# Sliding-window attention beside a dense network: attention blocks regrouped from six per stage in four stages to four per stage in six

## The chip, the cores and the metric

One core of a Trainium2 chip runs the whole program in one launch. The metric is the device time of that launch in microseconds (us), median of several executions. The engines are TensorE (PE in the profile, its weight loads PEld), VectorE (DVE), ScalarE (ACT), GpSimd (POOL) and the queue that issues most transfers, SyncE (SP). Each engine runs its instructions in order and waits on semaphores.

## What is computed

Three stages, cut to what matters:

```python
# q, k, v: (4, 8, 576, 64)   batch, heads, positions, head size
mask = (rel >= 0) & (rel < 64)               # each query sees 64 keys back
attn = softmax(where(mask, q @ k.T / 8, -1e9))
x = (attn @ v)                               # -> (2304, 512), rows by batch and position
h = ((x @ w1) * (x @ w2)) @ w3 @ w_out       # dense: 512 -> 1024 -> 1024 -> 512
e_idx = argmax(h @ w_gate)                   # one of 8 experts per row
out = gate * sigmoid(...) * relu(h @ ew1[e]) @ ew2[e]
```

## The kernel before, in words

Every large product is three products of fp32r parts: a high part and what the rounding left over (`product3`, L495 to L498: high x high, high x low, low x high). So each operand has a copy made by ScalarE (`h`) and a difference made by VectorE or GpSimd (`l`).

**Fold.** The kernel first multiplies w3 by w_out (and by the gates) into W, 512 + 16 columns, so that the dense part needs only w1, w2 and W. `w_order` lists its 16 tiles; the first two are done together in quarters. A W tile is 24 matmuls of 256 or 272 columns. Its result goes through ScalarE (`Wh`, L876) and VectorE (`Wl`, L1109). Beside that the fold splits w3 (`w3_steps`) and w1/w2 (`w12_steps`: at which tile each of eight pieces is copied by ScalarE; GpSimd makes the differences of the first six, L1463, and VectorE of the last two, `LATE`, L1065).

**Chunks.** The 2304 rows are six chunks of 384. `xTh` and `xTl` hold the transposed attention result of 1152 rows (two batches), three chunks. A chunk has 14 tiles, called steps e = 0 to 13: eight hidden tiles (w1 and w2, 24 matmuls of 384 columns) and six row tiles (24 matmuls against W, first three of 272 columns, then three of 256). The last chunk is followed by the routing and the experts, which the change leaves alone.

**Attention** has 24 blocks: a block is four heads by 192 queries (three groups of 64, each against 128 keys). They are put between the tiles of the stage before the chunk that needs them. A block passes through these pieces, each a function of the step after which it runs:
- `score` (TensorE, L587): 12 products into banks 5 and 7. It waits for q and k, and for the masks of the block before.
- `masks` (VectorE, `laid`): per head pair, scale and add the mask (L1021), take the maximum of two halves (L1025); then the row maximum (L1027).
- `exps` (ScalarE, `raised`, L830): six exponentials with sums.
- `weigh` (VectorE, `weighed`, L1045 and L1047) and `normal` (GpSimd, L1453): reciprocal, and the probabilities multiplied by it.
- `turn` (TensorE, `turned`, L599): three transposes into bank 4. It waits for `p_ok` of its block and for `pt_ok`, bank 4 read out for the block before.
- `turn_out` (VectorE, L1037): four copies out of bank 4, `pt_ok`.
- `value` (TensorE, `valued`, L612), `value_hi` (ScalarE, L835), `value_lo` (VectorE, L1051): product with v into bank 6, and its two parts into xTh and xTl. `value` waits for `o_lo`, the `value_lo` of the block before.

Before, a batch (six blocks) is done per stage, `NP` = 6, in four stages: in the fold, and in chunks 0, 2 and 3 (counted from 0); chunks 1, 4 and 5 have none. The blocks start every second step, and everything of one step runs in the order `turn`, `value`, `score` on TensorE. On VectorE, `weigh` stands inside the tile's own work, ahead of `turn_out`, `value_lo` and `masks` of the same step. The last block's `value` stands inside the last tile, behind nine of its matmuls:

```python
if b is not None and KF + i == NSTEP - 1:
    row_tile(i, n, tt, lambda: value(b, LAST))
```

**Transfers.** All loads are issued by the sync queue in an order written out by hand (up to L470). q and k of a block are two transfers into a buffer of a whole batch's two head pairs, v two more into tiles for even and odd starts. A load waits until the buffer's part was read (`next_qk`, `next_v`), and what stands behind it in the queue waits with it. Expert weights are loaded into the same room once the last block is done (`o_done`).

Of the kernel before, what the change touches and what calls it, by code (L numbers as in the profile page):

```python
# [18 lines left out]
P = 128  # L19
# [4 lines left out]
ALU = mybir.AluOpType  # L24
# [5 lines left out]
def build(nc, B, H, S, qT_in, kT_in, v_in, w1, w2, w3T_in, w_out, w_outT, w_gates, ew1, ew2, out):  # L30
    DM, FF = w1.shape
    D = DM // H
# [7 lines left out]
    SFULL = S // P  # L40
# [15 lines left out]
    UNITS = B * PAIRS  # L56
    UPS = 2 * PAIRS
# [7 lines left out]
    NP = PAIRS * NGRP // 2  # L65
    NSTEP = KF + 2 * CT
    assert 2 * NP + 2 == NSTEP and NCH == 3
# [4 lines left out]
    with ctx:  # L72
# [34 lines left out]
        put("raw_room", P)  # L107
# [110 lines left out]
        w12_hi, w12_lo, w1_lo = sem("w12_hi"), sem("w12_lo"), sem("w1_lo")  # L218

        qk_in, v_in_ok = [sem(f"qk_in{j}") for j in range(NGRP)], [sem(f"v_in{j}") for j in range(NGRP)]  # L220
# [15 lines left out]
        ew_hi, ew_lo = [sem("ew1_hi"), sem("ew2_hi")], [sem("ew1_lo"), sem("ew2_lo")]  # L236
# [15 lines left out]
        def v_tile(r, i):  # L252
            t = vA if key_start(i) % P == 0 else vB
            c = key_start(i) // P * 2 + r
            return t[:, c * P:(c + 1) * P]

        v_tiles = [[sorted({key_start(i) // P for i in range(3 * j, 3 * j + 3) if key_start(i) % P == odd * WIN})
                    for j in range(NGRP)] for odd in range(2)]
        unit_of = lambda p: divmod(p, NGRP)
# [41 lines left out]
        def pair_x(t, p, parity):  # L301
            u, j = unit_of(p)
            c = parity * S + j * 3 * WIN
            return t[:, :].rearrange("p (k c) -> p k c", c=SUPER)[:, 2 * u:2 * u + 2, c:c + 3 * WIN]
# [18 lines left out]
        def fold_scored(i):  # L323
            return i - 2 if i in (2, 3) else scored(i - 2) if i > 3 else None

        def fold_laid(i):
            return i - 2 if i in (2, 3) else laid(i - 2) if i > 3 else None

        def fold_raised(i):
            return 0 if i == 2 else raised(i - 2) if i > 3 else None  # L330

        def fold_weighed(i):
            return weighed(i - 2) if i > 2 else None
# [5 lines left out]
        w12_steps = [3, 6, 8, 10, 11, 12, 13, 14]  # L339
        LATE = 2 * KD - 2  # L340
# [43 lines left out]
        def _(sp):  # L384
# [33 lines left out]
            def load_qk(u, j):  # L418
                cols = slice(j * 3 * WIN, (j + 1) * 3 * WIN)
                for t, src in ((qT, qT_in), (kT, kT_in)):  # L420
                    sp.dma_start(t[:, :].rearrange("p (r s) -> p r s", s=S)[:, :, cols],
                                 src[bass.ds(u * 2, 2), :, cols].rearrange("r p s -> p r s")).then_inc(qk_in[j], 16)

            def load_v(u, j):
                for odd, vt in enumerate((vA, vB)):
                    t0, t1 = v_tiles[odd][j][0], v_tiles[odd][j][-1] + 1
                    sp.dma_start(vt[:, t0 * 2 * P:t1 * 2 * P].rearrange("p (t c) -> p t c", c=2 * P),
                                 v_in[bass.ds(u, 1), odd * WIN + t0 * P:odd * WIN + t1 * P, :].rearrange("o (t p) c -> p (o t) c", p=P)
                                 ).then_inc(v_in_ok[j], 16)

            def next_qk(u, j):
                sp.wait_ge(s_done, u * (2 * NGRP) - (2 * NGRP) + min(2 * j + 4, 2 * NGRP))
                load_qk(u, j)

            def next_v(u, j):
                sp.wait_ge(o_done, u * NGRP - NGRP + j + 1)
                load_v(u, j)

            load_qk(0, 0)
            for i in range(KF // 2):  # L440
                load_wo(1, i)
            load_qk(0, 1)
            load_qk(0, 2)
            load_v(0, 0)
            load_w12(0)
            load_v(0, 1)
            load_w12(1)
            load_v(0, 2)
            next_qk(1, 0)
            load_w3(4)  # L450
            next_qk(1, 1)
            next_qk(1, 2)
            load_w12(2)
            load_w3(6)
# [1124 lines left out]
```

## Time and profile before

| | |
|---|---|
| median of 3 runs | 717.49 us (716.71 to 718.61) |
| profiled execution, its own time | 718.94 us |
| its span, first to last instruction | 717.2 us |
| instructions | 15001 |
| mean granted clock of TensorE | 0.995 of full speed |
| busy VectorE, ScalarE, GpSimd | 378.0, 268.5, 119.9 us |
| q and k, each of 24 transfers of 192 KB | 3.0 and 4.0 us to landing |
| fold, chunks, and rest | to 84 us, to 437, to 717 |

The span is what the trace's rows add up to; the 1.7 us between it and the execution's time lie around it. In a timeline a row's second number is the duration of one instruction or of a merged group. TensorE's matmuls overlap, so the step from one to the next (start to start) is what counts there, and it is shorter than the duration. "idle before <-" names what ended an idle time.

### The profile page before, as it was taken

What the parts mean: (1) busy time and instruction counts of PE and PEld (TensorE: products, weight loads), DVE (VectorE), ACT (ScalarE), POOL (GpSimd) and SP (SyncE); (2) the same over time, 40 slices, a digit from 0 to 9 for tenths busy, and PEclk for the clock granted to TensorE, in tenths of its full rate; (3) what the DMA queues carried; (4) which work ended last, traced back from release to release, by engine and by line L of the source; (5) the groups of instructions that cost most, each with busy time, mean ns of one, the idle gap of its engine ahead of it and who ended that gap; (6) DMA issues with size and microseconds to landing.
All of it is one profiled execution on the core that took longest, in us unless ns stands there. A gap on an engine that the chain in (4) does not pass through costs nothing.

```text
span 717.2 us, 15001 instructions
## 1 busy us (share of the span) xinstructions
PE 701.5 (98%) x5075; PEld 639.1 (89%) x5076; DVE 378.0 (53%) x711; ACT 268.5 (37%) x651; POOL 119.9 (17%) x179
## 2 busy tenths in 40 slices
PE   8999899999999999999999999999999999999997
PEld 7999799999999989999999999878888888888885
DVE  5789657732237755782222568845356554662211
ACT  4466244322124324432211254444446444552121
POOL 7224200100010010001000001222222122222211
PEclk9999899999999999999999999999999999999999
DMA  9875121320012242115201043746265753511110
GB/s 328 273 263 175 45 67 39 111 82 1 4 64 60 66 138 75 29 36 199 81 1 45 1 127 126 262 161 216 75 224 187 234 173 133 183 35 44 32 44 30
DMA packets 44590, 80.12 MB, mean 112 GB/s; under 512 B 4413, under 2 KB 24893, under 8 KB 44544
## 3 DMA queue, kind: packets, MB, share of 16 engines
q1 hardware_dynamic: 39504, 64.01, 27.3%
q0 software_dynamic: 5040, 15.47, 6.2%
q8 instruction: 32, 0.52, 0.3%
q14 instruction: 14, 0.11, 0.0%
HBM read 70.03 MB, written 10.49 MB: 112 GB/s over the span
## 4 chain that ended last, share of the span: by engine, by line
PE 91%; DVE 4%; DMA 1%; issue 1%; ACT 1%; POOL 1%; POOLq 0%; DVEq 0%; ACTq 0%
PE bank L496 27%; PE bank L498 26%; PE bank L497 26%; PE bank L771 3%; PE bank L587 3%; PE bank L612 2%; DVE pT L1037 2%; PE bank L749 1%; PE bank L599 1%; DMA xs<-x_rows,gidc 1%; DVE prob L1025 1%; PE bank L509 1%; PE bank L731 1%; DMA w3r<-in_w3T 1%; DVE w3l L1058 1%
## 5 line engine op out<-in xcount | busy, mean ns | idle before, releaser
L496 PE MATMUL bank<-Wh,abh 128*128 128x272 f32 (+1 forms) x288 | 83.5, 290 | 0.0
L498 PE MATMUL bank<-Wh,abl 128*128 128x272 f32 (+1 forms) x288 | 82.1, 285 | 0.0
L1128 DVE TENSOR_TENSOR wbuf<-raw,wbuf 128x1024 f32 (+1 forms) x64 | 75.3, 1220 | 12.5 <-ACT wbuf L896 12.4
L497 PE MATMUL bank<-Wl,abh 128*128 128x272 f32 (+1 forms) x288 | 81.9, 284 | 0.0
L1329 DVE TENSOR_TENSOR hTl<-bank,hTh 128x512 fp32r<-128x512 f32 x44 | 28.4, 685 | 97.9 <-ACT hTh L944 90.5
L1149 DVE TENSOR_TENSOR ab_f<-bank,a_sb 128x384 f32<-128x384 f32 x48 | 26.7, 555 | 94.2 <-PE bank L498 93.7
L496 PE MATMUL bank<-wbuf,hTh 128*128 (+1 forms) x176 | 70.7, 402 | 0.6 <-issue 0.6
L496 PE MATMUL bank<-wbuf,xsTh 128*128 (+1 forms) x176 | 70.5, 400 | 0.0
L498 PE MATMUL bank<-wbuf,hTl 128*128 (+1 forms) x176 | 68.8, 391 | 0.0
L497 PE MATMUL bank<-wbuf,xsTh 128*128 (+1 forms) x176 | 68.7, 390 | 0.0
L498 PE MATMUL bank<-wbuf,xsTl 128*128 (+1 forms) x176 | 68.6, 390 | 0.0
L497 PE MATMUL bank<-wbuf,hTh 128*128 (+1 forms) x176 | 68.4, 389 | 0.0
L904 ACT ACTIVATE abh<-ab_f 128x384 fp32r<-128x384 f32 x48 | 25.2, 525 | 111.8 <-DVE ab_f L1149 111.8
L496 PE MATMUL bank<-xTh,w1h 128*128 128x384 f32 x192 | 66.0, 344 | 0.0
L497 PE MATMUL bank<-xTl,w1h 128*128 128x384 f32 x192 | 64.2, 335 | 0.0
L498 PE MATMUL bank<-xTh,w1l 128*128 128x384 f32 x192 | 64.2, 334 | 0.0
L498 PE MATMUL bank<-xTh,w2l 128*128 128x384 f32 x192 | 64.2, 334 | 0.0
L496 PE MATMUL bank<-xTh,w2h 128*128 128x384 f32 x192 | 64.1, 334 | 0.0
L497 PE MATMUL bank<-xTl,w2h 128*128 128x384 f32 x192 | 64.1, 334 | 0.0
L896 ACT ACTIVATE wbuf<-raw 128x1024 f32 (+1 forms) x64 | 63.9, 1054 | 0.0
L1037 DVE TENSOR_TENSOR pT<-bank,side 64x384 f32<-64x384 f32 x96 | 53.1, 554 | 12.7 <-PE bank L599 11.3
L496 PEld LDWEIGHTS bank<-Wh,abh 128*128 128x128 f32 x288 | 54.2, 188 | 1.1 <-issue 0.5
(218 smaller groups left out, 1479.9 us busy)
## 6 DMA issues: line engine op xcount, KB each, us to landing
raw<-in_expert_w SPq DMA_DIRECT2D x64, 512.0 KB, 4.4
qT<-in_qT SPq DMA_DIRECT2D x24, 192.0 KB, 3.0
kT<-in_kT SPq DMA_DIRECT2D x24, 192.0 KB, 4.0
x_rows<-x_sb POOLq DMA_DIRECT2D x18, 256.0 KB, 2.3
w3r<-in_w3T SPq DMA_DIRECT2D x8, 512.0 KB, 6.2
wo<-in_w_out SPq DMA_DIRECT2D x8, 256.0 KB, 8.0
woT<-in_w_outT SPq DMA_DIRECT2D x4, 512.0 KB, 8.3
vA<-in_v SPq DMA_DIRECT2D x16, 128.0 KB, 2.2
```

What stands on the lines that cost most here:

```text
L496: pe.matmul(dst, lh, rh, start=first, stop=False)
L497: pe.matmul(dst, lh, rl, start=False, stop=False)
L498: return pe.matmul(dst, ll, rh, start=False, stop=last)
L587: mm = pe.matmul(score_bank(h)[r * WIN:(r + 1) * WIN, (i % 3) * P:(i % 3 + 1) * P], qT[rows, r * S + i * WIN:r * S + (i + 1) * WIN], kT[ro ...
L612: mm = pe.matmul(bank[6][r * D:(r + 1) * D, (3 * h + i) * WIN:(3 * h + i + 1) * WIN], v_tile(r, 3 * j + i)[:, h * D:(h + 1) * D], pT[buf_o ...
L771: mm = pe.transpose(bank[3 + n][:, (f % 4) * P:(f % 4 + 1) * P], h_sb[:, f * P:(f + 1) * P], ident[:, :])
L896: act.activation(wbuf[:, bass.ds(wcol(e, part, 0, c * PC), PC)], raw[part * NP1 + c][:, :], ACT.Copy).then_inc(ew_hi[part], 1)
L904: act.activation(abh[:, f * CH:(f + 1) * CH], ab_f[f % 2][:, :], ACT.Copy).then_inc(ab_hi, 1)
L1037: cut = dve.tensor_tensor(pT[buf_of(p, h)][w * WIN:(w + 1) * WIN, :].rearrange("p (i r c) -> p i r c", r=2, c=WIN), bank[4][rows, 0:3 * P] ...
L1128: dve.tensor_tensor(wbuf[:, bass.ds(wcol(e, part, 1, c * PC), PC)], raw[part * NP1 + c][:, :], f32(wbuf[:, bass.ds(wcol(e, part, 0, c * PC ...
L1149: dve.tensor_tensor(ab_f[f % 2][:, :], hidden_bank(cc, f, 1)[:, 0:CH], a_sb[f % 2][:, :], ALU.mult).then_inc(ab_ok, 1)
L1329: dve.tensor_tensor(hTl[last][:, cols], bank[3 + n][:, :], f32(hTh[last][:, cols]), ALU.subtract).then_inc(hT_lo, 1)
```

## The change

The 24 blocks are ordered as the chunks need them: of each pair of batches, first the blocks of the first 384 rows (both halves of the heads), then of the next 384, then of the last. `NP` becomes 4, and every stage but the last chunk has attention: the fold and chunks 0 to 4. q and k of a block are one transfer of 448 KB, v one of 384 KB, each into one of two buffers by the block's parity; the host lays them out block by block (keys that two blocks share are stored twice). The steps at which pieces run are given as tables. In `masks` the two maxima are one instruction over both head pairs. Of the differences of w1 and w2, GpSimd now makes three (pieces 2, 4, 5) and VectorE five, and two of the steps at which they are copied change. The sync queue has no loop left for attention; in each stage it issues the loads of blocks two to five ahead.

```diff
+def pair_order(B, H):
+    order = []
+    for si in range(B // 2):
+        for stage in (((0, 0), (0, 1)), ((0, 2), (1, 0)), ((1, 1), (1, 2))):
+            order += [(2 * si + half, u, j) for u in range(H // 4) for half, j in stage]
+    return order
...
-    NP = PAIRS * NGRP // 2
+    PLACES = pair_order(B, H)
+    STAGES = NSUP * NCH
+    NP = len(PLACES) // STAGES
...
-        qT, kT = put("qT", 2 * S), put("kT", 2 * S)
-        vA, vB = put("vA", 2 * SFULL * P), put("vB", 2 * SFULL * P)
-        sm = put("sm", 3 * P)
+        qk = [put(f"qk{i}", QK) for i in range(2)]
+        vv = [put(f"vv{i}", 6 * P) for i in range(2)]
+        sm = put("sm", 2 * 3 * P)
...
         def scored(e):
-            return e // 2 + 1 if e % 2 == 0 and e // 2 + 1 < NP else None
+            return {2: 1, 5: 2, 8: 3}.get(e)
+
+        def laid(e):
+            return {0: 0, 3: 1, 6: 2, 9: 3}.get(e)
+
+        def raised(e):
+            return {1: 0, 4: 1, 7: 2, 9: 3}.get(e)
+
+        def weighed(e):
+            return {2: 0, 5: 1, 8: 2, 10: 3}.get(e)
 
         def turned(e):
-            return e // 2 - 1 if e % 2 == 0 and e >= 2 else None
+            return {4: 0, 7: 1, 10: 2, 11: 3}.get(e)
 
         def valued(e):
-            return e // 2 - 2 if e % 2 == 0 and e >= 4 else None
-
-        def laid(e):
-            return (e + 1) // 2 if e % 2 and (e + 1) // 2 < NP else None
-
-        def raised(e):
-            return e // 2 if e % 2 == 0 and e // 2 < NP else None
-
-        def weighed(e):
-            return e // 2 if e % 2 and e // 2 < NP else None
+            return {6: 0, 9: 1, 12: 2}.get(e)
...
-                batches = si * 2 + (1 if c == 0 else 2)
-                b = None if c == 1 or final else batches
-                chunk(cc, c, batches, b, 1 if c == 0 else 0, final)
+                chunk(cc, c, None if final else cc + 1, final)
...
         def fold_scored(i):
-            return i - 2 if i in (2, 3) else scored(i - 2) if i > 3 else None
+            return 0 if i == 2 else scored(i - 2)
...
-        w12_steps = [3, 6, 8, 10, 11, 12, 13, 14]
-        LATE = 2 * KD - 2
+        w12_steps = [3, 6, 8, 9, 10, 12, 13, 14]
+        w12_pool = (2, 4, 5)
...
+            def load_qk(G):
+                if G >= 2:
+                    sp.wait_ge(s_done, 2 * (G - 1))
+                sp.dma_start(qk[G % 2][:, :], qk_pairs[G]).then_inc(qk_in[G % 2], 16)
+
+            def load_v(G):
+                if G >= 2:
+                    sp.wait_ge(o_done, G - 1)
+                sp.dma_start(vv[G % 2][:, :], v_pairs[G]).then_inc(v_in[G % 2], 16)
+
+            load_qk(0)
             for i in range(KF // 2):
                 load_wo(1, i)
+            load_qk(1)
+            load_v(0)
             load_w12(0)
+            load_v(1)
+            load_qk(2)
             load_w12(1)
             load_w3(4)
+            load_qk(3)
+            load_w3(6)
             load_w12(2)
             load_w3(5)
             load_w12(3)
             load_w12(4)
+            load_qk(4)
             load_w12(5)
+            load_v(2)
+            load_w3(7)
             load_w12(6)
+            load_qk(5)
             load_w12(7)
+            load_v(3)
+            load_v(4)
+            load_v(5)
+            for G in range(NP, len(PLACES), NP):
+                for load, ahead in ((load_qk, 2), (load_qk, 3), (load_qk, 4), (load_v, 2),
+                                    (load_qk, 5), (load_v, 3), (load_v, 4), (load_v, 5)):
+                    if G + ahead < len(PLACES):
+                        load(G + ahead)
...
                 for h in range(2):
-                    g = 2 * G + h
-                    dve.wait_ge(s_done, g + 1)
-                    if g > 0:
-                        dve.wait_ge(laid_ok, g)
-                    dve.scalar_tensor_tensor(sm[:, :], score_bank(h)[:, 0:3 * P], SEQ_SCALE,
+                    dve.wait_ge(s_done, 2 * G + h + 1)
+                    dve.scalar_tensor_tensor(sm[:, h * 3 * P:(h + 1) * 3 * P], score_bank(h)[:, 0:3 * P], SEQ_SCALE,
...
-                    dve.wait_ge(masked, g + 1)
-                    dve.tensor_tensor(pr[:, :, h, :], smv[:, :, 0, :], smv[:, :, 1, :], ALU.max).then_inc(laid_ok, 1)
-                dve.wait_ge(laid_ok, 2 * G + 2)
+                dve.wait_ge(masked, 2 * G + 2)
+                smv = sm[:, :].rearrange("p (h i w c) -> p h i w c", h=2, w=2, c=WIN)
+                dve.tensor_tensor(prob[p % 2][:, :].rearrange("p (i h c) -> p h i c", h=2, c=WIN),
+                                  smv[:, :, :, 0, :], smv[:, :, :, 1, :], ALU.max).then_inc(laid_ok, 1)
+                dve.wait_ge(laid_ok, G + 1)
...
-                if b is not None:
-                    masks(b, 0)
                 for f in range(KF):
```

The last cut is in VectorE's `chunk`: block 0's masks stood ahead of the first hidden tile's work there and now follow it (`laid` of step 0).

## Rows read from the trace of the kernel before

**Rows 1.** The page, busy us of the engines (share of the span) and instructions.
```profile
PE 701.5 (98%) x5075; PEld 639.1 (89%) x5076; DVE 378.0 (53%) x711; ACT 268.5 (37%) x651; POOL 119.9 (17%) x179
```

**Rows 2.** The waits of TensorE: line, releaser, us in total, times, longest us.
```profile
PE bank L599 <- POOL prob L1453: 4.6, 4, 3.4
```

**Rows 3.** Windows by stage: us, busy us by engine, granted clock, DMA share, GB/s.
```profile
84.08:149.96 65.88, 64.84 (x644) 61.70 (x644) 43.68 (x96) 23.84 (x97) 6.25 (x8) 1.00 0.26 77
149.96:200.89 50.93, 50.93 (x339) 50.80 (x337) 10.44 (x22) 9.30 (x19) 1.62 (x3) 1.00 0.06 21
75.20:82.03 6.83, 6.14 (x61) 5.36 (x61) 2.97 (x6) 1.43 (x2) 0.54 (x1) 0.50 0.23 60
```

**Rows 4.** The timeline of TensorE, first chunk: start us, us, engine, line, operation.
```profile
120.82 0.44 PE L496 MATMUL bank<-xTh,w1h 128*128 128x384 f32 x1
...
123.00 0.33 PE L496 MATMUL bank<-xTh,w2h 128*128 128x384 f32 x1
...
125.08 0.28 PE L496 MATMUL bank<-Wh,abh 128*128 128x272 f32 x1
...
128.35 0.52 PE L599 MATMUL bank<-ident,prob 128*128 128x128 f32 x3
...
130.47 0.39 PE L496 MATMUL bank<-Wh,abh 128*128 128x272 f32 x1
...
136.62 0.49 PE L599 MATMUL bank<-ident,prob 128*128 128x128 f32 x3
137.04 0.45 PE L612 MATMUL bank<-pT,vA 128*64 128x64 f32 x8
...
137.89 0.39 PE L496 MATMUL bank<-Wh,abh 128*128 128x256 f32 x1
...
143.68 0.49 PE L599 MATMUL bank<-ident,prob 128*128 128x128 f32 x3
...
146.00 0.28 PE L498 MATMUL bank<-Wh,abl 128*128 128x256 f32 x1
...
147.22 0.28 PE L612 MATMUL bank<-pT,vB 128*64 128x64 f32 x2 [0.95 <-DVE xTl L1051]
```

**Rows 5.** The timeline of TensorE in the fold.
```profile
27.62 0.89 PE L587 MATMUL bank<-kT,qT 64*64 64x128 f32 x24
...
28.76 0.36 PE L496 MATMUL bank<-xTh,w3h 128*128 128x272 f32 x1 [0.25 <-DVE wol L1073]
```

**Rows 6.** The timeline of ScalarE, first chunk.
```profile
138.40 0.34 ACT L830 ACTIVATE prob<-prob,nmx 128x64 f32<-128x64 f32 x1
...
140.30 0.19 ACT L830 ACTIVATION_READ_ACCUMULATOR prob<-prob,nmx 128x1 f32 x1
...
145.07 0.49 ACT L835 ACTIVATE xTh<-bank 128x384 fp32r<-128x384 f32 x1 [0.80 <-PE bank L612]
```

**Rows 7.** The timeline of VectorE, first chunk.
```profile
86.65 0.36 DVE L1025 TENSOR_TENSOR prob<-sm 128x192 f32<-128x192 f32 x1
87.04 0.55 DVE L1027 TENSOR_REDUCE nmx<-prob 128x6 f32<-128x384 f32 x1
...
134.22 0.16 DVE L1045 TENSOR_SCALAR sums<-sums 128x6 f32<-128x6 f32 x1
...
134.52 0.53 DVE L1021 SCALAR_TENSOR_TENSOR sm<-bank,mask 128x384 f32<-128x384 f32 x1
...
140.52 0.17 DVE L1045 TENSOR_SCALAR sums<-sums 128x6 f32<-128x6 f32 x1
...
144.21 2.28 DVE L1037 TENSOR_TENSOR pT<-bank,side 64x384 f32<-64x384 f32 x4 [3.29 <-PE bank L599]
...
146.52 0.56 DVE L1051 TENSOR_TENSOR xTl<-bank,xTh 128x384 fp32r<-128x384 f32 x1
```

**Rows 8.** The timeline of VectorE in the fold.
```profile
65.82 1.76 DVE L1025 TENSOR_TENSOR prob<-sm 128x192 f32<-128x192 f32 x1
...
73.87 1.19 DVE L1065 TENSOR_TENSOR w1l<-w1r,w1h 128x1024 fp32r<-128x1024 f32 x1
```

More of the change, by code:

```diff
@@ L27, with build @@
 NEG = -1.0e30
-def build(nc, B, H, S, qT_in, kT_in, v_in, w1, w2, w3T_in, w_out, w_outT, w_gates, ew1, ew2, out):
+def pair_order(B, H):
[4 more added lines that the diff above has]
+    return order
+def build(nc, B, H, S, qk_pairs, v_pairs, w1, w2, w3T_in, w_out, w_outT, w_gates, ew1, ew2, out):
     DM, FF = w1.shape
@@ L106, in build @@
         mask, side = put("mask", 4 * P), put("side", 2 * 4 * WIN)
-        put("raw_room", P)
+        put("raw_room", 6 * P)
         attn_end = put.o
@@ L250, in key_start, with key_offset @@
             return WIN * max(i - 1, 0)
[L252 to L259, printed above, removed]
+        def key_offset(j, i):
+            return key_start(3 * j + i) - key_start(3 * j)
+        head_of_row = lambda G: PLACES[G][2] == 0
         score_bank = lambda h: bank[5 + 2 * h]
@@ L323, in fold_scored @@
         def fold_scored(i):
-            return i - 2 if i in (2, 3) else scored(i - 2) if i > 3 else None
[L326 to L333, printed above, removed]
+            return 0 if i == 2 else scored(i - 2)
         w3_steps = {1: 3, 5: 4, 7: 5, 9: 6, 11: 7}
-        w12_steps = [3, 6, 8, 10, 11, 12, 13, 14]
-        LATE = 2 * KD - 2
+        w12_steps = [3, 6, 8, 9, 10, 12, 13, 14]
+        w12_pool = (2, 4, 5)
+        pool_count = lambda n: sum(i in w12_pool for i in range(n))
         assert len(w12_steps) == 2 * KD
@@ L463, in _ @@
             load_w12(7)
-            next_v(1, 2)
-            with sp.Fori(2, UNITS // 2) as u:
-                for j in range(NGRP):
-                    next_qk(u, j)
-                for j in range(NGRP):
-                    next_v(u, j)
+            load_v(3)
[6 more added lines that the diff above has]
+                        load(G + ahead)
@@ L578, in score @@
                 G = b * NP + p
-                u, j = unit_of(p)
-                pe.wait_ge(qk_in[j], (b * (PAIRS // 2) + u + 1) * (16 * 2))
+                j, buf = PLACES[G][2], qk[G % 2]
+                pe.wait_ge(qk_in[G % 2], 16 * (G // 2 + 1))
                 if G > 0:
                     pe.wait_ge(masked, 2 * G)
-                for i in range(3 * j, 3 * j + 3):
+                for i in range(3):
                     for h in range(2):
@@ L887, in _ @@
                     hi_wo(1)
-                if fold_raised(i) is not None:
-                    exps(0, fold_raised(i))
+                if raised(i - 2) is not None:
+                    exps(0, raised(i - 2))
                 if i in w12_steps:
@@ L1032, in turn_out @@
                 rows = slice(h * WIN, (h + 1) * WIN)
-                lead = 0 if unit_of(p)[1] == 0 else 1
+                lead = 0 if head_of_row(G) else 1
                 dve.wait_ge(pt_done, G + 1)
@@ L1109, in own @@
                     dve.tensor_tensor(Wl[:, ws], w_bank(i)[:, 0:end - first], f32(Wh[:, ws]), ALU.subtract).then_inc(W_lo, 1)
-                    if fold_weighed(i) is not None:
-                        weigh(0, fold_weighed(i))
+                    if weighed(i - 2) is not None:
+                        weigh(0, weighed(i - 2))
                 if i == len(w_order) - 1:
-                    value_lo(0, LAST, 0)
+                    value_lo(0, LAST)
                 own()
@@ L1119, in _ @@
                 if i >= 2 and valued(i - 2) is not None:
-                    value_lo(0, valued(i - 2), 0)
-                if fold_laid(i) is not None:
-                    masks(0, fold_laid(i))
+                    value_lo(0, valued(i - 2))
+                if laid(i - 2) is not None:
+                    masks(0, laid(i - 2))
             weight_splits(len(w_order) - 1)
@@ L1180, in chunk @@
                     if b is not None and KF + i == NSTEP - 1:
-                        value_lo(b, LAST, parity)
+                        value_lo(b, LAST)
                     row_tile(i, n, tt)
@@ L1462, in lo_w12 @@
                 pool.wait_ge(w12_hi, i + 1)
-                pool.tensor_tensor(wl[:, ws], wr[:, ws], f32(wh[:, ws]), ALU.subtract).then_inc(w12_lo, 1)
+                pool.tensor_tensor(wl[:, ws], wr[:, ws], f32(wh[:, ws]), ALU.subtract).then_inc(w12_lo_pool, 1)
             for i in range(len(w_order)):
-                if fold_weighed(i) is not None:
-                    normal(0, fold_weighed(i))
-                if i in w12_steps[:LATE]:
+                if weighed(i - 2) is not None:
+                    normal(0, weighed(i - 2))
+                if i in w12_steps and w12_steps.index(i) in w12_pool:
                     lo_w12(w12_steps.index(i))
```

120 lines of the change are left out of this document (44 added, 76 removed).

## The prediction

> **What bounds the kernel now.** I read the page's busy times first: TensorE is busy 701.5 us of a span of 717.2 [rows 1]. Whatever the change does to other engines counts only through TensorE: how much it has to issue, where it waits, and at which clock it runs. Then the waits of TensorE: four waits of `turn` (L599) for GpSimd's normalisation, 4.6 us in all, the longest 3.4 [rows 2]; all lie in the fold, where attention runs between the products of w3 and w_out. Then the windows by stage [rows 3]. A chunk without attention takes 50.93 us and TensorE has no idle time in it; the chunk with six blocks takes 65.88. VectorE is busy 43.68 us in the one and 10.44 in the other, so a block costs VectorE about 5.5 us, and the DMA engines are at 0.26. The third window, just behind the 3.4 us wait, has a granted clock of 0.50, that is 1.2 GHz in place of 2.4, with TensorE busy for 6.14 us of it.
>
> Last, TensorE's own timeline through a chunk with attention [rows 4]. Start to start, the twelve matmuls of w1 behind a `score` take 2.18 us and the next twelve 2.08: the first piece behind attention costs 0.10 more. Two row tiles of 272 columns take 6.15 us behind attention, so 3.03 each plus 0.10 once; two of 256 columns take 5.79, so 2.85 each plus 0.10. A `turn` takes 0.42 us, a `value` 0.85. The first row tile takes 3.27, with 0.25 more than it needs, spent on the normalisation. The last `value` starts 1.22 us behind the ninth matmul of its tile where 0.12 is the step: 1.1 us of waiting.
>
> **Part 1: attention is spread over six stages of four blocks.** All 24 blocks remain, with the same matmuls, so their own time only moves (two blocks out of the fold, two out of each chunk that had six, four into each that had none). What changes is the number of places at which tiles are interrupted. By the schedule functions a stage has 9 such places before (start, after 0, 2, 4, 6, 8, 10, 12, and inside the last tile), in four stages: 36. After, it has 12 (start, after 2, 4, 5, 6, 7, 8, 9, 10, 11, 12, inside the last), in six stages: 72. At 0.10 us each, 36 more add **3.6 us**; the bounds are 0, should the step hide behind weight loads, and 0.13.
>
> In the fold, `score` 1 no longer stands behind the fourth tile. Before, it ran at 27.62 and TensorE then waited 0.25 us for the low part of the gate columns until 28.76 [rows 5]. Nothing stands in its place, so all of that 1.1 us is idle: **+0.85 us**, since the block's work comes later anyway.
>
> **Part 2: the waits that go.** `weighed` and `turned` are now two tiles apart for blocks 0 to 2 where they were one, so normalisation is done long before it is asked for: the four fold waits go, **-4.6** [rows 2], and with the longest the half clock behind it, 6.14/2 = **-3.1** [rows 3]. In three chunks the 0.25 us behind the first row tile go, **-0.75**, and the wait of the last `value`, 3 x 1.1 = **-3.3** [rows 4], because no `turn_out` stands before `value_lo` any more. What remains of it: `value` 3 needs the low half of `value` 2, which is 0.97 us from the start of a `value` to ScalarE's copy (144.10, which is `turn` at 143.68 and 0.42, to 145.07), 0.52 for the copy, 0.56 for the subtraction and 0.14 to TensorE (147.08 to 147.22) [rows 4, 6, 7], together 2.19, against 0.85 + 0.10 + 9 x 0.119 = 2.02 of TensorE's work: 0.17 us in five chunks, **+0.85**.
>
> **Part 3: the new wait.** Block 3 is the tight one. Its mask is made after tile 9, its exponentials follow, its sums are taken after tile 10, block 2 is turned out only behind them on VectorE, and `turn` 3 on TensorE after tile 11 waits until block 2 is out of bank 4. Before, two turns stood two tiles apart; now these two are one apart.
> From the end of tile 9, TensorE has `value` 1 0.85, tile 10 3.13, `turn` 2 0.42, tile 11 2.95: 7.35 us.
> The other chain: 0.97 and 0.52 as above; `value_lo` 0.50; the masks, now two scale-and-mask steps, one maximum over 384 columns and one reduction; 0.03 to ScalarE; the exponentials 2.12 (138.40 to 140.52); sums and reciprocal 0.30 (134.22 to 134.52); `turn_out` 2.28 and 0.14 to TensorE [rows 6, 7]. The masks I put at 0.53 + 0.53 for the two steps, 0.56 and 0.55 for maximum and reduction with 0.03 before each, 2.2 in all: the wide maximum is in no row, 192 columns take 0.36 and two of these 0.72, I take 0.56. Sum 9.1 us, a wait of **1.75 us**, 1.55 to 1.9 by those bounds. Queued behind the waiting `weigh` on VectorE is nothing but this `turn_out`. Five chunks: **+8.8**.
> In the fold the same chain holds one more copy on ScalarE and one more subtraction on VectorE, of tile 12, each narrower than the 0.49 and 0.56 of 384 columns [rows 6, 7]: 0.4 each. A w1 split on GpSimd can lie beside the maximum; in the fold a maximum beside one took 1.76 us in place of 0.36 [rows 7, 8], so 0 to 1.4 more, and I take 0.2, as they meet only at the edge. That makes 2.7 us there (2.3 to 4.1): **+2.7**.
>
> **Part 4: what I cost at nothing.** Three of six splits of w1/w2 go from GpSimd to VectorE, 3 x 1.2 us of VectorE [rows 8], against two blocks fewer, 2 x 5.5 us [rows 3]: the fold's VectorE is freer than before, and only a backlog longer than a tile would reach TensorE. The merged maxima shorten VectorE's masks; they are in the chain above and nowhere else. The two transfers of a block are 448 and 384 KB, in place of 384 and 256 to 384. On the sync queue each load waits for the block two before it and is asked for at least three tiles later, over 9 us. Load 2 now stands before w2's second piece, load 3 before w3's seventh, load 4 and `v` 2 before later pieces of w1: each wait ends on a block that TensorE has done three or more tiles before the piece is due. With the DMA engines at 0.26 in a chunk this is covered; if the cover fails, TensorE stands for the whole missing part. The expert weights' first loads wait for block 24, now at the end of the fifth chunk, and are needed behind the eight hidden tiles of the sixth, 33 us on.
>
> **Sum.** Gone: 4.6 + 3.1 + 3.3 + 0.75 = 11.7. New: 3.6 + 0.85 + 0.85 + 8.8 + 2.7 = 16.8. Net +5.1 us on the span of 717.2. The profiled execution itself took 718.94, 1.45 above the median of 717.49; I add the difference to the median: **722.6 us**. The largest single gain, 7.7 us in the fold, is real, and is paid back because one wait now comes six times.
>
> **Rivals.** (a) The fold's new wait brings the clock down. A wait of 3.4 us did so before, ones of 1.1 did not [rows 2 to 4]; 2.7 lies between. Price 3.1 us: 725.7, slower still. Chance 0.17; against it, the point estimate is below the one wait that did it. The Trainium skill, "TensorE: Matmul & The Clock Gate", section "Why this matters for your kernels", warns that idle gaps between bursts of matmuls bring the half clock back; by it this rival is the danger of any schedule with one long wait, and the trace agrees with its 6.14 us at 0.50.
> (b) Not slower: block 3's chain closes in time. If it reaches TensorE within 7.35 us after tile 9, the 8.8 and 2.7 vanish: 711.1. It needs 1.75 us out of ScalarE's exponentials and VectorE's order, for instance if `turn_out` 2 ran before `weigh` 3. The code gives weights first, so 0.10.
> (c) The waits are there, but the interruptions cost nothing and the wait is at its lower bound: 722.6 - 3.6 - 1.0 = 718.0, no change. 0.12.
> (d) A load comes late in the fold, or VectorE's backlog reaches TensorE there: 3 to 5 us more, 727. 0.08.
> The forecast itself: 0.53.
>
> **How the numbers follow.** A measurement tells 0.3% from nothing, that is 2.2 us. Faster is (b); same is (c); slower is the forecast, (a) and (d). The range from 718 to 727.5 leaves out (b) and part of (d).
>
> **What would show it.** TensorE's waits should list `turn` behind VectorE's `turn_out`, six times, about 1.7 us each and one near 2.7, and none behind GpSimd. Chunks one to five should each take about 50.93 + 4 x 2.09 + 1.2 + 1.9 = 62.4 us, where 2.09 is a block's own matmuls (0.42, 0.85 and some 0.82 of a `score`, whose 0.89 overlaps the next [rows 5]). The fold should end about 8 us earlier. I am wrong if the chunks take 60.5 (the wait is hidden), or if the granted clock shows a dip in each chunk, or if a DMA is named in TensorE's waits.

## The result, and the profile after

The changed kernel takes 724.88 us (median of four, 723.52 to 725.88) against 717.71 for the kernel before beside it: a ratio of 1.0099, interval 1.0077 to 1.0121. It is slower, inside the forecast range of 718 to 727.5 and 2.3 us above the forecast.

The page of the kernel after, head and busy row, answers to [rows 1]:

```profile
span 721.8 us, 14724 instructions
...
PE 702.3 (97%) x5075; PEld 638.6 (88%) x5076; DVE 368.0 (51%) x690; ACT 268.2 (37%) x651; POOL 113.6 (16%) x176
```

VectorE and GpSimd have 10.0 and 6.3 us less to do than in [rows 1], TensorE 0.8 more, and the span is 4.6 us longer. So 3.8 us of it were lost while TensorE stood, and 0.8 while it worked. Its waits, where [rows 2] had GpSimd's normalisation (line 583 is now `turn`, 1016 `turn_out`):

```profile
engine line waited for: us in total, times, longest us
PE bank L583 <- DVE pT L1016: 10.8, 6, 2.7
PE bank L557 <- DVE prob L1060: 1.5, 1, 1.5
PE bank L479 <- DVE wol L1052: 1.1, 1, 1.1
```

The waits for GpSimd are gone and so are the three of the last `value` for its low half. In their place stands one new kind, six times: `turn` for `turn_out` of the block before, 2.7 us in the fold and 1.6 in each of five chunks. The third line is the gate columns' wait: 1.1 us with nothing before it, where [rows 5] had 0.25. No DMA is in the list.

Windows of the kernel after (us, busy us by engine, granted clock, DMA share, GB/s, as in [rows 3]): the first, second and fifth chunk, and the stretch behind the fold's wait:

```profile
77.26:139.72 62.46, 60.81 (x542) 58.09 (x541) 31.30 (x68) 19.01 (x71) 4.66 (x6) 1.00 0.21 62
139.72:202.18 62.46, 60.82 (x542) 58.10 (x541) 30.61 (x66) 19.00 (x71) 4.99 (x7) 1.00 0.23 68
327.10:389.42 62.32, 60.67 (x541) 58.09 (x541) 30.61 (x66) 19.00 (x71) 4.98 (x7) 1.00 0.16 49
...
67.60:70.90 3.30, 3.30 (x18) 3.30 (x16) 2.88 (x6) 0.00 (x0) 0.69 (x1) 0.50 0.02 5
```

All five chunks with attention take 62.3 to 62.5 us, of which 1.65 is TensorE idle (62.46 less 60.81). The first chunk begins at 77.26 where it began at 84.08: the fold gains 6.8. The sixth begins at 389.42; before, chunks of 65.88 and 50.93 brought it there at 383.53, so the chunks lose 12.7 (312.16 against 299.45). What follows takes 332.4 against 333.6: there the profile of the kernel before has two waits of TensorE that this one has not, 0.6 us at 468.25 with no releaser in the profile and 0.4 at 467.01 for the gathered rows. The three make up the span: -6.8 + 12.7 - 1.3 = +4.6. The two rows of the kernel before:

```profile
467.01 0.66 PE L749 MATMUL bank<-ident,xs 128*128 128x128 f32 x4 [0.36 <-DMA xs<-x_rows,gidc]
468.25 0.49 PE L496 MATMUL bank<-wbuf,hTh 128*128 x1 [0.58 <-issue]
```

One wait in TensorE's timeline, first chunk after the change (columns as in [rows 4]): the tile after `turn` 2, and the wait at `turn` 3:

```profile
126.43 0.49 PE L583 MATMUL bank<-ident,prob 128*128 128x128 f32 x3
126.68 0.36 PE L479 MATMUL bank<-Wh,abh 128*128 128x256 f32 x1
...
129.49 0.28 PE L481 MATMUL bank<-Wh,abl 128*128 128x256 f32 x1
131.40 0.55 PE L583 MATMUL bank<-ident,prob 128*128 128x128 f32 x3 [1.63 <-DVE pT L1016]
```

From the tile's last matmul to the `turn` is 1.91 us where one step is 0.12: TensorE loses 1.79. What it waits for, in VectorE's timeline of the same stretch:

```profile
123.95 0.56 DVE L1030 TENSOR_TENSOR xTl<-bank,xTh 128x384 fp32r<-128x384 f32 x1 [0.88 <-ACT xTh L817]
124.43 1.01 DVE L998 SCALAR_TENSOR_TENSOR sm<-bank,mask 128x384 f32<-128x384 f32 x2
125.47 0.56 DVE L1003 TENSOR_TENSOR prob<-sm 128x384 f32<-128x384 f32 x1
126.07 0.55 DVE L1006 TENSOR_REDUCE nmx<-prob 128x6 f32<-128x384 f32 x1
...
128.79 0.17 DVE L1024 TENSOR_SCALAR sums<-sums 128x6 f32<-128x6 f32 x1 [1.65 <-ACT prob L812]
128.99 0.19 DVE L1026 RECIPROCAL rec<-sums 128x6 f32<-128x6 f32 x1
129.10 2.24 DVE L1016 TENSOR_TENSOR pT<-bank,side 64x384 f32<-64x384 f32 x4
```

`turn` 2 is in the bank at 126.9, and VectorE is idle for 1.65 us until 128.79, yet `turn_out` 2 starts only at 129.10: ahead of it in VectorE's order stands `weigh` 3, which waits for block 3's exponentials, and these for the masks made after tile 9. That is the chain of part 3 of the prediction. The wide maximum, which no row showed before, takes 0.56.

### The profile page after: what moved, and what is told of

The parts are those of the page before. It is cut to its first block, busy times and chain, and to the rows that moved or that the text cites. A ratio compares the mean times of both kernels' runs of the same rounds, so it can differ in the third digit from the quotient of the medians.

```text
span 721.8 us, 14724 instructions
## 1 busy us (share of the span) xinstructions
PE 702.3 (97%) x5075; PEld 638.6 (88%) x5076; DVE 368.0 (51%) x690; ACT 268.2 (37%) x651; POOL 113.6 (16%) x176
## 4 chain that ended last, share of the span: by engine, by line
PE 91%; DVE 5%; ACT 2%; issue 1%; DMA 1%; POOLq 0%; ACTq 0%; DVEq 0%
PE bank L479 27%; PE bank L481 25%; PE bank L480 25%; PE bank L595 3%; PE bank L571 3%; PE bank L753 3%; DVE pT L1016 2%; ACT prob L812 2%; PE bank L731 1%; PE bank L583 1%; DVE sm L998 1%; PE bank L492 1%; DVE prob L1003 1%; PE bank L713 1%; DMA w3r<-in_w3T 1%
## 5 line engine op out<-in xcount | busy, mean ns | idle before, releaser
L479 PE MATMUL bank<-Wh,abh 128*128 128x272 f32 (+1 forms) x288 | 85.4, 297 | 0.0
L1430 POOL TENSOR_TENSOR prob<-prob,rec 128x384 f32<-128x384 f32 x24 | 20.8, 867 | 286.6 <-DVE rec L1026 286.6
```

The costliest lines, as they stand in the source:

```text
L479: pe.matmul(dst, lh, rh, start=first, stop=False)
L1430: pool.tensor_tensor(pv, pv, rec[:, stats(p)].unsqueeze(2).broadcast_to([P, 6, WIN]), ALU.mult).then_inc(p_ok, 1)
```

## The experiments

All were timed beside the kernel before (717.2 to 718.2 us in their sessions) on one core. To compare two of them, take the difference of their ratios; 0.1% is 0.7 us. They add lines to the program, so the same code has other line numbers in some of them.

| kernel | us | ratio to before | interval |
|---|---|---|---|
| the change | 724.88 | 1.0099 | 1.0077 to 1.0121 |
| chunks_block3_early | 716.30 | 0.9983 | 0.9973 to 0.9994 |
| fold_retimed | 718.58 | 1.0015 | 1.0005 to 1.0024 |
| turn_out_first | 721.01 | 1.0051 | 1.0032 to 1.0071 |
| fold_wait_filled | 722.64 | 1.0076 | 1.0059 to 1.0093 |
| chunks_grouped | 713.79 | 0.9952 | 0.9934 to 0.9969 |
| best | 707.72 | 0.9871 | 0.9849 to 0.9893 |
| before_three_splits_moved | 717.91 | 1.0005 | 0.9995 to 1.0015 |
| two_maxima | 725.32 | 1.0114 | 1.0097 to 1.0131 |
| loads_twice | 724.17 | 1.0086 | 1.0070 to 1.0103 |
| gpsimd_six_splits | 723.84 | 1.0077 | 1.0060 to 1.0094 |

### Block 3 one tile earlier in the chunks

The fold keeps the change's tables; the chunks get:

```diff
 def scored(e):
-    return {2: 1, 5: 2, 8: 3}.get(e)
+    return {2: 1, 5: 2, 7: 3}.get(e)
 def laid(e):
-    return {0: 0, 3: 1, 6: 2, 9: 3}.get(e)
+    return {0: 0, 3: 1, 6: 2, 8: 3}.get(e)
 def raised(e):
-    return {1: 0, 4: 1, 7: 2, 9: 3}.get(e)
+    return {1: 0, 4: 1, 7: 2, 8: 3}.get(e)
```

> The changed kernel, with block 3's score, masks and exponentials one step earlier in the five chunks (score after step 7, masks and exponentials after step 8) and the fold left as it is. Theory (the wait of turn 3 for bank 4 is what the change costs): turn_out 2 is then ready before TensorE has done tile 11, the wait of 1.8 us goes in all five chunks, each chunk takes 60.6 us in place of 62.45, and the time falls by 9 us, to 715.9 (from 724.9, the kernel before at 717.7). Rival (the twelve interruptions of every stage cost it, not the wait): their number stays at twelve, and the time stays at 724 to 725. The fold's wait of 2.7 us stays under both.

716.30 us. Waits and first chunk of this kernel:

```profile
PE bank L589 <- DVE pT L1027: 2.7, 1, 2.7
```
```profile
78.51:139.19 60.68, 60.67 (x541) 58.06 (x540) 31.17 (x68) 18.87 (x71) 4.65 (x6) 1.00 0.20 65
```

The five short waits are gone and the fold's is left. A chunk takes 60.68, so 1.78 less, and TensorE is busy for all of it. Three table entries are worth 1.16%, more than the whole loss: without the wait of `turn` 3 in the chunks the change would not have been slower. One thing more differs: with `score` 3 behind `turn` 1 a chunk has eleven places of interruption and not the twelve that the expectation speaks of; by the prediction's price that is 0.1 us of the 1.78.

### VectorE's order at that place

```diff
 def weights(e):
-    if b is not None and weighed(e) is not None:
+    if b is not None and weighed(e) is not None and e != 10:
         weigh(b, weighed(e))
 def attend(e):
     if b is not None and turned(e) is not None:
         turn_out(b, turned(e), 0)
         turn_out(b, turned(e), 1)
+    if b is not None and e == 10:
+        weigh(b, weighed(e))
```

> The changed kernel; in the chunks VectorE turns block 2 out of bank 4 before it takes block 3's sums at step 10, nothing else. Theory: bank 4 is free 3.1 us after tile 10 ends and TensorE needs it at 3.4, so the wait for bank 4 goes; in its place the normalisation of block 3 comes late by some 0.9 us, since its sums now follow turn_out. The wait shrinks from 1.8 to about 0.9 us and changes its releaser from VectorE to GpSimd: 4 us faster, 721. Rival (the exponentials alone set the wait, whatever the order on VectorE): no change, 724.9.

721.01 us. Waits of this kernel, the two of `turn`:

```profile
PE bank L583 <- POOL prob L1432: 5.2, 5, 1.0
...
PE bank L583 <- DVE pT L1016: 2.7, 1, 2.7
```

With `turn_out` 2 ahead, bank 4 is free in time, and `turn` 3 waits 1.0 us for its own probabilities instead: a chunk takes 61.85, 0.6 less. So VectorE's order was the last link, but block 3's chain through exponentials, sums and normalisation is late by itself. So rival (b)'s remedy gives back a third of a chunk's 1.78 us, and the earlier block 3 all of it.

### The fold

The same idea in the fold alone, chunks as changed. It also puts `score` 1 back behind the gate columns' tile:

```diff
-            return 0 if i == 2 else scored(i - 2)
+            return 0 if i == 2 else {1: 1, 4: 2, 6: 3}.get(i - 2)
+fold_laid = {0: 0, 2: 1, 5: 2, 6: 3}.get
+fold_raised = {2: 0, 4: 1, 5: 2, 8: 3}.get
+fold_weighed = {2: 0, 5: 1, 7: 2, 8: 3}.get
+fold_turned = {4: 0, 6: 1, 10: 2, 11: 3}.get
+fold_valued = {6: 0, 10: 1, 11: 2}.get
```

> The changed kernel with the fold's steps retimed and the chunks left as they are: blocks 1 to 3 are scored one or two steps earlier (block 1 again behind the fourth tile, where it hides the wait for the gate columns), the sums of block 3 are taken at step 8. Theory: both fold waits (1.1 for the gates, 2.7 for bank 4) go, and with the second the half clock behind it. By durations alone the fold ends 4.1 us earlier; without the half clock 1.7 us more for a stretch of 3.4 us at 1.2 GHz, 3.4 us more for one of 6.8. Time 718 to 719.5. Rival: the half clock has another cause, then only 4.1 us go (720.8) and a stretch at 0.5 stays in the fold. The chunks' five waits of 1.8 us stay under both.

718.58 us, 0.84% below the change. Waits of this kernel, and its fold as one window:

```profile
PE bank L589 <- DVE pT L1027: 8.1, 5, 1.6
```
```profile
0.00:71.42 71.42, 69.27 (x661) 64.27 (x662) 48.35 (x87) 37.54 (x99) 26.97 (x51) 1.00 0.67 248
```

Only the chunks' five waits are left, there is no half clock in the fold, and it ends at 71.42 in place of 77.26. The 5.8 us are the 2.9 by which the wait holds TensorE up (below), some 0.9 of the gate columns', 1.7 of half clock (below) and 0.4 more. These tables also interrupt the fold at seven places where the change's do at twelve; at the prediction's 0.10 that would be 0.5, an estimate that no run takes apart.

### The half clock behind the fold's wait

TensorE's timeline in the fold after the change, at the wait:

```profile
64.28 0.28 PE L481 MATMUL bank<-xTl,w3l 128*128 128x272 f32 x1
67.28 0.71 PE L583 MATMUL bank<-ident,prob 128*128 128x128 f32 x3 [2.71 <-DVE pT L1016]
67.64 0.56 PE L479 MATMUL bank<-xTh,w3h 128*128 128x256 f32 x1
...
70.77 0.37 PE L481 MATMUL bank<-xTl,w3l 128*128 128x256 f32 x1
70.97 0.29 PE L479 MATMUL bank<-xTl,w3h 128*128 128x256 f32 x1
...
72.14 0.92 PE L595 MATMUL bank<-pT,vv 128*64 128x64 f32 x24
```

Behind 2.7 us of idleness a matmul of 256 columns takes 0.41 us in place of 0.28 until 70.8, at a granted clock of 0.50 (the last window above), 1.2 GHz in place of 2.4. The tile lasts 4.50 us (67.64 to 72.14) where its like lasts 2.93 (126.68 to 129.61 in the first chunk): with 0.12 in the `turn` 1.7 us are lost. The wait itself holds TensorE up for 2.88 us, 64.28 to 67.28 less a step of 0.12. Rival (a) happened, at half its price. To separate the idleness from the work behind it, this kernel fills the wait, with no result used:

```diff
 def turn(b, p):
+    if G == 3:
+        pe.wait_ge(masked, 8)
+        for _ in range(16):
+            pe.matmul(bank[7][:, 0:P], ident[:, :], ident[:, :], start=True, stop=True)
```

> The changed kernel with 16 extra matmuls (identity by identity, 128 columns, into bank 7, their result is read by nobody) put ahead of turn 3 in the fold, so that TensorE works through most of its wait of 2.7 us. No work of the reference is changed. Theory (the idle wait brings the half clock): no stretch at 0.5 in the fold, the extra matmuls cost nothing, the time falls by 1.7 to 3.4 us, to 721.5 to 723.2. Rival (the half clock comes from elsewhere or costs nothing): the stretch stays and the time is 724.9 or more.

722.64 us, by the ratios 0.23% below the change. The intervals of the two overlap, so the times alone do not settle it; the granted clock does. Two windows of its profiled execution, an early stretch and the one behind `turn` 3:

```profile
28.32:31.74 3.42, 2.95 (x13) 2.98 (x14) 1.07 (x5) 2.86 (x13) 0.00 (x0) 0.50 0.02 5
67.00:72.00 5.00, 5.00 (x46) 5.00 (x45) 4.05 (x8) 0.94 (x1) 2.77 (x2) 1.00 0.01 3
```

Behind `turn` 3 the clock stays at 1.00. The three executions beside this one ran at a mean clock of 0.999, which leaves some 2 us of half clock at most in the whole program, so no stretch of 3.4 us (worked out from span and mean clock). All seven profiles of the changed fold in which the wait was left idle have it. So it was the idleness. But this execution has a half clock that I did not expect, right behind the gate columns' wait of 1.1 us, and it was the slowest of its four (724.36; the others 722.54 to 722.68, so about 1.7 us for the stretch, as above). chunks_block3_early (28.16 to 31.57) and two_maxima (29.62 to 33.03) show the same stretch; the profile of the change, with the same wait, does not.

### What freed the fold: the schedule or the lighter GpSimd

The kernel before, with pieces 2, 4 and 5 of the w1/w2 differences on GpSimd and five on VectorE, and nothing else:

```diff
-        LATE = 2 * KD - 2
+        w12_pool = (2, 4, 5)
...
-                if i in w12_steps[LATE:]:
+                if i in w12_steps and w12_steps.index(i) not in w12_pool:
```

> The kernel before, six blocks per stage, with one part of the change alone: of the differences of w1 and w2, GpSimd makes pieces 2, 4 and 5 and VectorE the other five. It asks what freed the fold: the schedule (normalisation is asked for two tiles later) or GpSimd's lighter load. Theory (the schedule): the four waits of turn for the normalisation stay, since normalisation is still asked for one tile after the sums, and with them the half clock: 716.5 to 718.5, no change; the longest wait may shrink from 3.4 us to some 2.2 because GpSimd has one split less ahead of it, and VectorE's 3 x 1.2 us are covered. Rival (the split beside it made them): the waits fall to under 1 us in all and the half clock goes, 710.5 to 712.

717.91 us, 1.0005: no change. Waits of this kernel, and the window behind the longest:

```profile
PE bank L600 <- POOL prob L1453: 4.4, 3, 3.4
PE bank L613 <- DVE xTl L1051: 2.8, 3, 0.9
```
```profile
75.73:79.15 3.42, 3.29 (x31) 2.87 (x32) 2.29 (x5) 0.89 (x2) 0.00 (x0) 0.51 0.00 0
```

One wait less, the longest still 3.4 and the half clock still behind it, 3.42 us of it where the profile of before had 6.83. So it was not the splits but the new schedule that freed the fold; that it was the two tiles between `weighed` and `turned` is argued from the code and was not tried alone. The other way round, the change with GpSimd's six splits back:

```diff
-        w12_pool = (2, 4, 5)
+        w12_pool = (0, 1, 2, 3, 4, 5)
```

> The changed kernel with the first six differences of w1 and w2 on GpSimd again and two on VectorE, as before the change; all else as changed. Theory (a split of GpSimd beside VectorE's masks slows them, and the fold's turn 3 hangs on those masks): the fold's wait of turn 3 grows from 2.7 us to some 3.5, the chunks stay at 62.4, and the half clock behind it lasts longer: 725.5 to 727.5. Rival (the work taken off GpSimd did nothing): 724.9, wait 2.7.

723.84 us, not above the change. The mechanism is there, the price is not. Waits and VectorE's maximum in its fold, then the same maximum in the fold of the change:

```profile
PE bank L583 <- DVE pT L1016: 11.4, 6, 3.3
...
60.29 1.60 DVE L1003 TENSOR_TENSOR prob<-sm 128x384 f32<-128x384 f32 x1
```
```profile
60.32 1.00 DVE L1003 TENSOR_TENSOR prob<-sm 128x384 f32<-128x384 f32 x1
```

GpSimd's split lies beside the maximum for 1.18 us here (until 61.47) and for 0.59 in the change (until 60.91). The maximum runs 0.6 us longer and the wait is 0.6 longer. In this profile the half clock began at 67.33 (window below), half a microsecond before `turn` 3 was let go at 67.85: what of it falls into the wait costs nothing, so the tile behind took 4.06 us in place of 4.50. Moving three splits was worth nothing in either kernel.

```profile
67.33:70.74 3.41, 2.89 (x14) 2.89 (x15) 2.79 (x6) 0.00 (x0) 1.54 (x1) 0.50 0.00 0
```

### The merged maxima and the transfers

The maximum head pair by head pair again:

```diff
-                dve.wait_ge(masked, 2 * G + 2)
-                dve.tensor_tensor(prob[p % 2][:, :].rearrange("p (i h c) -> p h i c", h=2, c=WIN),
-                                  smv[:, :, :, 0, :], smv[:, :, :, 1, :], ALU.max).then_inc(laid_ok, 1)
+                for h in range(2):
+                    dve.wait_ge(masked, 2 * G + h + 1)
+                    dve.tensor_tensor(pr[:, h], smv[:, h, :, 0, :], smv[:, h, :, 1, :], ALU.max).then_inc(laid_ok, 1)
```

> The changed kernel with the maximum of a block made head pair by head pair again, 192 columns each, in place of one over 384. It leads to the exponentials of block 3 on the chain that sets turn 3. Before, 192 columns took 0.36 us. In the chunks VectorE has the second pair's scores as soon as the first, so two of them take 0.72 + a gap where one takes 0.56 to 0.7: theory (the chain through the masks sets turn 3): every wait of turn 3 grows by 0.1 to 0.3 us, 725.5 to 726.5, and the waits of TensorE at turn rise from 13.5 us to 14.1 to 15.3. Rival (masks are not on that chain): unchanged at 724.9, waits unchanged at 13.5.

725.32 us, 0.15% above, inside both intervals. The waits of `turn`, and VectorE at block 3 in its first chunk:

```profile
PE bank L583 <- DVE pT L1017: 10.7, 6, 2.9
```
```profile
126.22 1.01 DVE L998 SCALAR_TENSOR_TENSOR sm<-bank,mask 128x384 f32<-128x384 f32 x2
127.15 0.62 DVE L1005 TENSOR_TENSOR prob<-sm 128x192 f32<-128x192 f32 x2
127.81 0.55 DVE L1007 TENSOR_REDUCE nmx<-prob 128x6 f32<-128x384 f32 x1
```

My expectation failed. Two narrow maxima take 0.62 and not 0.72 plus a gap. From the first mask step to the reduction is 1.59 us here (126.22 to 127.81) and 1.64 with one wide maximum (124.43 to 126.07). A chunk takes 62.40 against 62.46. Merging gives nothing. That masks are on the chain stands by the experiment before: there the fold's wait grew by what the maximum did. It did here too: in the fold the two narrow ones take 1.25 us beside the split where the wide one took 1.00, and the wait is 2.9.

Every load of blocks 6 to 23 made twice, the second after the first has landed:

```diff
 sp.dma_start(qk[G % 2][:, :], qk_pairs[G]).then_inc(qk_in[G % 2], 16)
+if G >= 6:
+    sp.wait_ge(qk_in[G % 2], 16 * (2 * (G // 2) - 2))
+    sp.dma_start(qk[G % 2][:, :], qk_pairs[G]).then_inc(qk_in[G % 2], 16)
```

> The changed kernel with every load of q and k and of v for blocks 6 to 23 made twice into the same buffer, the second issued when the first has landed. TensorE waits for the second. A load is so twice as many bytes and comes a landing time later (3.2 us for q and k, 3.5 for v in the changed kernel's trace), and the queue stands for that time. Theory (the loads of the chunks are hidden; a load has three tiles, over 9 us, of room): 724.9 within 0.8, no DMA in TensorE's waits. Rival (the room is used up, the transfers are part of the time): each block late by a few tenths to 3 us, 730 or more, with waits of TensorE for a DMA at the score or the value in each chunk.

724.17 us, the same as the change. Its second chunk, to be held against the window 139.72:202.18 above:

```profile
140.42:202.86 62.44, 60.81 (x545) 58.09 (x541) 30.60 (x66) 18.98 (x71) 4.98 (x8) 1.00 0.39 122
```

The DMA share goes from 0.23 to 0.39 and the chunk stays at 62.4, with no DMA in TensorE's waits. The loads of the chunks are hidden with at least one landing time to spare. This says nothing of the loads of the fold, which were left as they were.

### Fewer places, and both together

The early block 3 with its pieces put between fewer tiles, first alone, then with the retimed fold:

```diff
 def turned(e):
-    return {4: 0, 7: 1, 10: 2, 11: 3}.get(e)
+    return {5: 0, 7: 1, 10: 2, 11: 3}.get(e)
 def valued(e):
-    return {6: 0, 9: 1, 12: 2}.get(e)
+    return {7: 0, 10: 1, 11: 2}.get(e)
```

> The chunks of chunks_block3_early, with the same pieces put between fewer tiles: turn 0 moves from behind tile 4 to behind tile 5 (where score 2 is), value 0 behind tile 7 (with turn 1 and score 3), value 1 behind tile 10 (with turn 2), value 2 behind tile 11 (with turn 3). A chunk has 7 places at which its tiles are interrupted in place of 11; the work is the same and the fold is untouched. Theory (an interruption costs 0.10 us, and the last value waits 0.17 us for the low half of the block before): 5 x 4 x 0.10 + 5 x 0.17 = 2.85 us less than chunks_block3_early's 716.3, so 713.4, and chunks of 60.1 to 60.2 us in place of 60.7. Rival (the time belongs to the pieces and not to the places, so grouping them gives nothing): 715.5 to 716.3, chunks of 60.5 to 60.7. A wait of a turn for a value's bank or of a value for its operands would add to either and would show in TensorE's waits.

> The chunks of chunks_grouped and the fold of fold_retimed together. If the gains add: the changed kernel's 724.9, less 8.6 for block 3 earlier in the chunks, 2.9 for grouping, and 6.3 for the fold (724.9 - 718.6) = 707.1. Rival (the fold and the chunks are coupled: block 4's load and masks, or the state in which the fold leaves VectorE, take back part of it): 709 to 711, with a wait of TensorE in the first chunk or for a DMA. By the theory the fold keeps five short waits of turn of about 1.6 us and the chunks have none over 0.3.

713.79 and 707.72 us. The first chunk of chunks_grouped, then waits and first chunk of best:

```profile
77.28:137.52 60.24, 60.24 (x541) 58.03 (x541) 31.14 (x68) 19.10 (x71) 4.66 (x6) 1.00 0.19 65
```
```profile
PE bank L563 <- DVE prob L1071: 1.5, 1, 1.5
PE bank L531 <- DVE wol L1063: 0.9, 1, 0.9
...
72.29:132.54 60.25, 60.25 (x544) 58.04 (x540) 30.62 (x67) 19.09 (x71) 4.69 (x7) 1.00 0.19 67
```

Grouping gives 0.44 us a chunk, where I expected 0.57. The wait of the last `value` had less than the expected 0.17 us to give: that `value` starts 0.29 behind the last matmul in chunks_block3_early (136.11 to 136.40) and 0.21 here (134.51 to 134.72), as any `value` does that waits for nothing. So 0.08 is the wait and four places fewer give 0.36, near the 0.40 expected. In best no `turn`, `value` or `score` is left among TensorE's waits. One line of its expectation was wrong by my own slip: it said the fold would keep five waits of 1.6 us, but those lay in the chunks and are gone with them. The gains add: 724.88, less 8.6, 2.5 and 6.3 for the three steps, is 707.5, and 707.72 was measured. This version beats both kernels, the one before by 1.3% (0.9849 to 0.9893).

## Why the prediction was right, by its steps

**What bounds it.** TensorE does: VectorE has ten us less to do and the kernel is slower, by TensorE's waits, its clock and its interruptions.

**The new wait (+8.8 in the chunks, +2.7 in the fold).** This step decided, and its chain holds the right links: 1.79 us measured for 1.75, and 2.88 for 2.7. Taking it away in the chunks brought 8.6 us back. That the size came out so near is in part luck. The chain took 8.94 us (122.46 to 131.40), not 9.1 (the terms as written add up to 9.06), as `turn_out` and the way from it to TensorE were 0.12 shorter; TensorE's own work beside it took 7.15, not 7.35, mostly because a `turn` that stands alone takes 0.25 us and not 0.42. The two errors cancel. In the fold the maximum took 1.00 us, not 0.56 and the 0.2 allowed for the split beside it; the other terms of the chain came out shorter, 9.98 us in all for 10.1, and TensorE's own work took 7.10.

**What went.** The 4.6 us of waits for GpSimd went, and before_three_splits_moved and gpsimd_six_splits show that it was by the schedule. So did the 0.25 us behind the first row tile: `turn` 1 now stands ahead of that tile, and it lasts 3.19 (115.23 to 118.42) with both its places, where it took 3.27. The last `value`'s 3.3 went too; by the forecast's measure 0.18 us of it is left (136.91 in the first chunk, 0.30 behind the last matmul, less a step of 0.12), forecast at 0.17. Half of that is no wait: a `value` that waits for nothing starts 0.21 behind the last matmul (134.50 to 134.71).

**The half clock (-3.1).** This is the term that failed. I let it go whole; 3.4 us of it came back behind the 2.7 us wait, and rival (a), to which I gave 0.17, is what happened, with 1.7 us lost and not 3.1. It is also why the fold ends 6.8 us earlier and not about 8. My argument against it, that 2.7 lies below the one wait that had done it, was no argument: the nearest row on the other side was at 1.1, and a wait of 1.1 too, that of the gate columns, is followed by the half clock in some executions. The Trainium skill, "TensorE: Matmul & The Clock Gate", section "Why this matters for your kernels", names idle gaps between bursts of matmuls as what drops the clock; the filled wait, with 1.00 behind it, agrees.

**The interruptions (+3.6).** The size of a chunk was right, and four places grouped away gave 0.36 us for 0.40. But the places are not alike. A chunk of the change has 1.2 us beyond matmuls and waits (62.46 - 50.93 - 4 x 2.09 - 1.79 - 0.18): I took 12 places at 0.10. Four of the twelve hold a `turn` alone, and such a one takes 0.25 (126.43 to 126.68) and not the 0.42 that I had counted in the 2.09, which pays for the place. Eight places at 0.15 fit 62.46 and seven at 0.14 fit 60.24. This division is fitted to two chunks; no run takes it apart. By it the term is 6 x 1.2 less 4 x 1.06 (what the chunk of 65.88 leaves), +3.0.

**The gate columns (+0.85).** As forecast: 1.1 us idle. **Costed at nothing:** the chunks' loads, the splits and the maxima, each tried, each nothing; the fold's loads were not tried, and no DMA is in TensorE's waits. So rival (d) didn't happen; (c), interruptions for nothing, is refuted by the grouping.

**The sum.** +5.1 forecast on the span, +4.6 in the two profiled executions: half clock +1.7, the part after the fifth chunk -1.3, which I had at nothing, interruptions -0.6, and -0.3 is left. These terms offset each other, so the near sum is in part luck. Of the -1.3, 1.0 are the two waits that the profile of before has there and that of the change has not; in the experiments this part takes 332.4 to 333.3 us, most where a wait of 0.6 without a releaser stands in it again, so it belongs to the execution and not to the change. The medians differ by 7.2 because the profiled execution of before lay 1.2 us above its median (718.94) and that of after was its fastest (723.52), 1.4 below. The four executions of the change have spans of 721.8, 722.7, 723.6 and 724.1 at mean clocks of 0.996, 0.996, 0.994 and 0.993: 0.003 of 722 is 2.2 us, about the whole spread. The mean also takes in some 2 to 3 us of half clock at the very end, where TensorE has no work (2.3 in the profile); what the means of 0.993 and 0.994 need beyond that is more than one stretch of 3.41. So the half clock lasts longer in the slower ones, by this estimate, which the single profile did not show. The ten executions of chunks_block3_early show the same: 714.95 to 715.72 us at 0.997, 716.28 to 717.22 at 0.994 and 0.995. My transfer from one execution to the median was blind to that.

## What to carry to other kernels

When pieces of a pipeline are moved apart to hide one wait, look for the two that end up nearest together, and add up both chains between them from rows: here one pair was a tile apart, and its wait came six times. A wait on a shared bank is often set by what stands ahead of the bank's reader in that engine's order; but moving the reader alone uncovers the chain behind it, so start the late block earlier. A wait in front of dense matmuls can have a second price, the half clock behind it: here one of 2.7 us or more had it in every profile, one of 1.1 in three of eight, and it varies between executions.

## What the runs showed of the hardware

- While TensorE had work, a stretch of half clock lasted 3.41 us in the change and in eight experiments (two of them had two such), and 6.83 in the kernel before. In the profiles it followed every fold wait of 2.7 us or more that was left idle, nine of nine. It never followed the chunks' waits of 1.6 us idle, of which five stand in each of six profiles, nor the five of 1.0 in turn_out_first. Yet it followed the 1.1 us of the gate columns in three of the eight profiles that have it. That wait lies only 20 us behind the idleness of the start. What decides there stays open.
- It isn't in every execution: one of turn_out_first ran at a mean clock of 1.000 and took 719.57, against 720.92 to 721.80 for the other three. One of the kernel before ran at 1.000 too and took 717.63, no less than that kernel's median, so other things vary by as much. In the profiles of fold_retimed and best, where no wait in the fold behind its first 16 us is over 0.3 us, it doesn't occur.
- Where the stretch began before the wait was over, the part inside the wait cost nothing (gpsimd_six_splits: begun at 67.33, TensorE let go at 67.85, the tile behind 0.4 us shorter than in the change).
- VectorE's maximum over 384 columns took 0.56 us alone, 1.00 where GpSimd's split lay beside it for 0.59 us, and 1.60 where it did for 1.18; over 192 columns, two took 0.62 in sequence.
- Three transposes took 0.25 us ahead of a tile's matmuls and 0.42 ahead of a `score` or `value`.
